# Attention, two MLPs and Sinkhorn on one core: 1/|p|^2 transposed instead of conj(p)/|p|^2, with the order around it

## The reference

```python
scale = np.minimum(mag, 0.999) / (mag + 1e-06)
new_re = ar * S_re - ai * S_im
new_im = ar * S_im + ai * S_re
S_re, S_im = (new_re + k_t outer v_t, new_im)
y_t = q_t @ S_re
```

## Time and profile before

| what | value |
|---|---|
| median of 3 runs | 2314.96 us (2314.71 to 2316.58) |
| the profiled execution, its own time | 2314.06 us |
| its span, first to last instruction | 2312.3 us |
| TensorE busy | 2228.5 us (96%) |
| VectorE busy | 1736.3 us (75%) |
| ScalarE busy | 1000.8 us (43%) |
| GpSimd busy | 506.5 us (22%) |
| mean granted TensorE clock | 0.990 |

### The profile page before, as it was taken

One profiled execution on the slowest core, in us unless ns is written; L12 is line 12 of the kernel. 1 busy time (PEld: TensorE's weight loads), 2 busy tenths in 40 slices (PEclk: granted clock), 3 DMA queues, 4 the chain that ended last, 5 costly groups with the idle time before them and its releaser, 6 DMA issues.

```text
span 2312.3 us, 38147 instructions
## 1 busy us (share of the span) xinstructions
PE 2228.5 (96%) x13735; PEld 2080.2 (90%) x13735; DVE 1736.3 (75%) x3033; ACT 1000.8 (43%) x1689; POOL 506.5 (22%) x332
## 2 busy tenths in 40 slices
PE   3799999999998989999999999999999999999999
PEld 2799999999998889999998899999998999999998
DVE  7888888888855777677777777777778777776775
ACT  3565666556555424333344333443334333344332
POOL 0000000000000333222332223322323223332222
PEclk9899999999999999999999999999999999999999
DMA  4211111111103121111011230111111211011111
GB/s 122 83 49 50 53 50 49 50 50 49 43 29 123 42 82 56 55 55 55 31 51 55 83 107 30 55 55 55 55 42 41 82 56 55 29 53 54 54 55 28
DMA packets 70726, 131.34 MB, mean 57 GB/s; under 512 B 5512, under 2 KB 36488, under 8 KB 70536
## 3 DMA queue, kind: packets, MB, share of 16 engines
q1 hardware_dynamic: 70536, 129.14, 17.2%
HBM read 114.96 MB, written 14.16 MB: 56 GB/s over the span
## 4 chain that ended last, share of the span: by engine, by line
PE 88%; DVE 8%; issue 1%; ACT 1%; DMA 0%; POOL 0%; SPq 0%; DVEq 0%; ACTq 0%
PE bank L1536 15%; PE bank L1537 15%; PE bank L1538 15%; PE bank L1701 11%; PE bank L1702 11%; PE bank L1703 11%; PE bank L1485 2%; PE bank L1504 2%; PE bank L1514 2%; PE bank L1513 2%; PE bank L1471 1%; PE bank L1523 1%; DVE tmp L923 1%; DVE u_s L1319 1%; DVE x_raw L1215 0%
## 5 line engine op out<-in xcount | busy, mean ns | idle before, releaser
L1701 PE MATMUL bank<-w_h,h_h 128*128 128x384 f32 x1536 | 516.0, 336 | 11.2 <-DVE acc L1345 6.8
L1703 PE MATMUL bank<-w_h,h_l 128*128 128x384 f32 x1536 | 514.1, 335 | 0.0
L1702 PE MATMUL bank<-w_l,h_h 128*128 128x384 f32 x1536 | 514.0, 335 | 0.0
L597 POOL TENSOR_TENSOR h_l<-u_s,h_h 128x512 fp32r<-128x512 f32 x192 | 245.1, 1298 | 974.8 <-ACT h_h L830 974.8
L1537 PE MATMUL bank<-x_l,w_h 128*128 128x512 f32 x1056 | 414.4, 392 | 0.0
L1536 PE MATMUL bank<-x_h,w_h 128*128 128x512 f32 x1056 | 414.2, 392 | 0.0
L1538 PE MATMUL bank<-x_h,w_l 128*128 128x512 f32 x1056 | 413.3, 391 | 0.0
L1345 DVE SCALAR_TENSOR_TENSOR acc<-bank,prob,acc 128x384 f32<-128x384 f32 x352 | 214.5, 612 | 174.2 <-PE bank L1703 171.5
L1701 PEld LDWEIGHTS bank<-w_h,h_h 128*128 128x128 f32 x1536 | 288.9, 188 | 17.2 <-DVE acc L1345 10.0
L1702 PEld LDWEIGHTS bank<-w_l,h_h 128*128 128x128 f32 x1536 | 288.9, 188 | 2.0
L1703 PEld LDWEIGHTS bank<-w_h,h_l 128*128 128x128 f32 x1536 | 288.8, 188 | 0.0
(11 more groups left out here) (176 smaller groups left out, 4133.6 us busy)
## 6 DMA issues: line engine op xcount, KB each, us to landing
...
```

The lines of the kernel that those rows point to most:

```text
L597: pool.tensor_tensor(tiles_of(h_l, name), group_sum(name), tiles_of(h_h, name).bitcast(F32), ALU.subtract).then_inc(hl_done, 1)
L1701: pe.matmul(dst, h_h[:, f, t_], w2h[:, fw], start=n == 0, stop=False)
L1702: pe.matmul(dst, h_h[:, f, t_], w2l[:, fw], start=False, stop=False)
L1703: mm = pe.matmul(dst, h_l[:, f, t_], w2h[:, fw], start=False, stop=n == 3)
```

## The change

Instead of p * rr, two parts, the kernel now takes `rr` alone to tokens: `r_by_tokens` has the small product and three transposes, into att[2]. On DVE `k_by_r` multiplies the transposed rr by k into the new tile `kr` and `by_k` multiplies kr by the transposed p, which stays in att[0] and att[1]. `pre_inv` (POOL) and `first_inv` (DVE) go. In odd units `r_by_tokens` stands directly behind `p_by_tokens`, ahead of `tile_in(t)`; in even units it stays behind `tile_in(t)`. The banks are passed round: q's transposes go to att[3] and att[2], k's to att[0] and att[1], the scores to att[3] and att[2], y to att[0]. `ACT.p_root` now waits for `r_there`, `state_sum` always follows `y_sum`, `ysum` has two columns so that ACT may run one unit ahead, and SP loads the next k after `k_by_r`. In the tail, x2_hi and x2_lo of the last group but one move ahead of `g_hi` / `g_lo` of round m = 2, the first expert's weight work moves from rounds 1 and 2 to rounds 2 and 3, and TensorE runs the first expert's first product `p1_0` ahead of the last `mm_out`.

```diff
@@ -59,7 +59,7 @@
 R_MAX = 2.0 ** 80
-R_ONE = 2.0 ** 60
+R_ONE, R_HALF = 2.0 ** 60, 2.0 ** 30
 P2_MIN = 2.0 ** -93
@@ -125,7 +125,7 @@
         yr = sb("yr", [128, KT, 128], F32, ab)
-        ysum = sb("ysum", [128, 1], F32, ab)
+        ysum = sb("ysum", [128, 2], F32, ab)
         an = sb("an", [128, 2, NI, BKJ], F32, ab)
@@ -134,7 +134,7 @@
         rr = sb("rr", [128, KT, 128], F32, ab)
-        pinv = sb("pinv", [128, 2, KT, 128], F32, ab)
+        kr = sb("kr", [128, DM], F32, ab)
         qb = sb("qb", [128, DM], F32, ab)
@@ -149,7 +149,7 @@
         prod = tmp2[:].rearrange("p r k t -> p (r k t)")[:, 0:4 * BKJ].rearrange("p (q r n) -> p q r n", q=2, r=2)
-        mask_rows = pinv[:, 0, 0]
+        mask_rows = kr[:, 0:128]
@@ -331,7 +332,7 @@
                 if u:
-                    sp.wait_ge(k_mul, 2 * u)
+                    sp.wait_ge(kr_done, u)
                 sp.dma_start(kb[:], permuted(k[u // B, u % B])).then_inc(k_in, 16)
@@ -484,12 +485,6 @@
             pool.memset(inv_b[:], -1.0).then_inc(filled, 1)
-            def pre_inv(u):
-                pool.wait_ge(r_done, u + 1)
-                pool.wait_ge(i_there, 2 * u)
-                pool.tensor_tensor(pinv[:], p[:], rr[:].unsqueeze(1).to_broadcast([128, 2, KT, 128]), ALU.mult)\
-                    .then_inc(pinv_done, 1)
@@ -574,8 +569,6 @@
                 check_y(u)
-                if 2 <= u + 1 < UNITS:
-                    pre_inv(u + 1)
@@ -641,9 +634,9 @@
-                if u:
-                    act.wait_ge(floor_done, u)
-                act.activation(sq[:, 1], yr_u[:], ACT.Square, scale=2.0 ** -22, accum_out=ysum[:]).then_inc(ysq_done, 1)
+                if u > 1:
+                    act.wait_ge(floor_done, u - 1)
+                act.activation(sq[:, 1], yr_u[:], ACT.Square, scale=2.0 ** -22, accum_out=ysum[:, u % 2:u % 2 + 1]).then_inc(ysq_done, 1)
@@ -652,23 +645,23 @@
                 if u:
-                    act.wait_ge(pinv_done, u)
+                    act.wait_ge(r_there, u)
                     act.wait_ge(last_done, u)
...
             def stacks(u, half):
-                there, done, dst = ((qt_there, qs_done, qs), (kt_there, ks_done, ks))[half]
+                there, done, dst, from_ = ((qt_there, qs_done, qs, (3, 2)), (kt_there, ks_done, ks, (0, 1)))[half]
                 for n in range(2):
...
                     act.activation(dst[0:96, 4 * n:4 * n + 4],
-                                   att[2 * half + n][0:96, :].rearrange("p (h t) -> p h t", h=4), ACT.Copy)\
+                                   att[from_[n]][0:96, :].rearrange("p (h t) -> p h t", h=4), ACT.Copy)\
                        .then_inc(done, 1)
...
                 act.wait_ge(y_there, u + 1)
-                act.activation(y, att[2][:, 0:DM], ACT.Copy).then_inc(y_done, 1)
+                act.activation(y, att[0][:, 0:DM], ACT.Copy).then_inc(y_done, 1)
@@ -798,13 +791,15 @@
                 t = (GROUPS - 1) * TILES + m
+                if m == 2:
+                    x2_hi(GROUPS - 2)
                 g_hi(t - 1)
...
                 if m == 2:
-                    x2_hi(GROUPS - 2)
-                if m == 1:
-                    for part in range(3):
-                        w1_hi(0, 0, 0, part)
+                    w1_hi(0, 0, 0, 0)
+                    w1_hi(0, 0, 0, 1)
+                if m == 3:
+                    w1_hi(0, 0, 0, 2)
                 if m == 6:
@@ -907,7 +902,7 @@
                    .then_inc(scaling, 1)
-                dve.tensor_scalar(r_last[:, u % 4, KT:KT + 1], ysum[:], 2.0 ** 64, None, ALU.mult).then_inc(floor_done, 1)
+                dve.tensor_scalar(r_last[:, u % 4, KT:KT + 1], ysum[:, u % 2:u % 2 + 1], 2.0 ** 64, None, ALU.mult).then_inc(floor_done, 1)
                 dve.wait_ge(scaling, n + 3)
@@ -982,7 +977,6 @@
                     dve.wait_ge(p_there, 2 * u)
-                    dve.wait_ge(pinv_done, u)
                 dve.tensor_tensor(p[:, 0], tmp2[:, 0], tmp2[:, 1], ALU.subtract).then_inc(final_step, 1)
@@ -1006,18 +1000,8 @@
-            def first_inv(u):
-                dve.wait_ge(r_done, u + 1)
-                if u:
-                    dve.wait_ge(i_there, 2 * u)
-                else:
-                    dve.wait_ge(mask_done, 1)
-                dve.tensor_tensor(pinv[:], p[:], rr[:].unsqueeze(1).to_broadcast([128, 2, KT, 128]), ALU.mult)\
-                   .then_inc(pinv_done, 1)
             def bound(u):
-                dve.wait_ge(i_there, 2 * u + 1)
+                dve.wait_ge(r_there, u + 1)
                 dve.tensor_reduce(r_sum[0:1, u:u + 1], att[2][0:1, DM:DM + KT + 1], AX.X, ALU.add).then_inc(bound_done, 1)
@@ -1027,26 +1011,30 @@
-            def by_k(u, parts=(0, 1)):
+            def k_by_r(u):
+                bound(u)
                 dve.wait_ge(k_in, 16 * (u + 1))
-                for n in parts:
-                    if n == 0:
-                        bound(u)
-                    dve.wait_ge(i_there, 2 * u + n + 1)
-                    dve.scalar_tensor_tensor(kt[:, :, n], att[2 + n][:, 0:DM].rearrange("p (h d) -> p h d", h=H), -R_ONE,
-                                             kb[:].rearrange("p (h d) -> p h d", h=H), ALU.mult, ALU.mult)\
+                if u == 0:
+                    dve.wait_ge(mask_done, 1)
+                dve.scalar_tensor_tensor(kr[:], att[2][:, 0:DM], -R_HALF, kb[:], ALU.mult, ALU.mult).then_inc(kr_done, 1)
+            def by_k(u):
+                dve.wait_ge(kr_done, u + 1)
+                for n in range(2):
+                    dve.scalar_tensor_tensor(kt[:, :, n], att[n][:, 0:DM].rearrange("p (h d) -> p h d", h=H), R_HALF,
+                                             kr[:].rearrange("p (h d) -> p h d", h=H), ALU.mult, ALU.mult)\
                        .then_inc(k_mul, 1)
...
                     dve.wait_ge(s_there, 2 * u + n + 1)
-                    dve.tensor_tensor(at[:, 4 * n:4 * n + 4], att[n][:].rearrange("p (h t) -> p h t", h=4),
+                    dve.tensor_tensor(at[:, 4 * n:4 * n + 4], att[3 - n][:].rearrange("p (h t) -> p h t", h=4),
                                       mask[:].unsqueeze(1).to_broadcast([128, 4, 128]), ALU.mult).then_inc(at_done, 1)
...
                 dve.wait_ge(st_there, u + 1)
-                dve.wait_ge(y_there, u + 1)
                 dve.tensor_tensor(state[0:96, b, 0:DM], att[3][0:96, 0:DM], state[0:96, b, 0:DM], ALU.add)\
@@ -1088,16 +1076,14 @@
                 p_inv(0)
-                first_inv(0)
                 scale_sum(2)
-                by_k(0, (0,))
+                k_by_r(0)
+                by_k(0)
                 final(1)
-                by_k(0, (1,))
                 p_sum(1)
...
                 p_inv(1)
-                first_inv(1)
                 scale_sum(3)
@@ -1106,9 +1092,10 @@
                 by_q(1)
-                blocks(1, 1, 3)
+                blocks(1, 1, 2)
+                k_by_r(1)
                 by_k(1)
-                blocks(1, 3, NI)
+                blocks(1, 2, NI)
                 masked(1)
@@ -1150,6 +1137,7 @@
                     blocks(pair, BLOCKS_AHEAD, BLOCKS_AHEAD + 1)
+                k_by_r(u)
                 by_k(u)
@@ -1281,15 +1269,15 @@
                 t = (GROUPS - 1) * TILES + m
-                g_lo(t - 1)
                 if m == 2:
                     x2_lo(GROUPS - 2)
+                g_lo(t - 1)
                 if m == 5:
...
                 g_max(t)
-                if m == 1:
+                if m == 2:
                     w1_sums(0, 0, 0)
-                if m == 2:
+                if m == 3:
                     w1_lo(0, 0)
@@ -1454,46 +1442,45 @@
         def _(pe):
-            def to_tokens(u, src, done, first_bank):
+            def p_by_tokens(u):
+                pe.wait_ge(p_done, u + 1)
                 for n in range(2):
-                    if first_bank == 2 and n == 0:
-                        if u:
-                            pe.wait_ge(xl_done, u)
-                        pe.wait_ge(last_done, u + 1)
-                        pe.wait_ge(floor_done, u + 1)
-                        pe.matmul(att[2][:, DM:DM + KT + 1], ones[:], r_last[:, u % 4], start=True, stop=True)
-                    if first_bank == 2 and n == 1 and u:
-                        pe.wait_ge(state_done, u)
                     for kk in range(KT):
-                        mm = pe.transpose(att[first_bank + n][:, kk * 128:(kk + 1) * 128], src[:, n, kk], ident[:])
-                    mm.then_inc(done, 1)
-            def p_by_tokens(u):
-                pe.wait_ge(p_done, u + 1)
-                to_tokens(u, p, p_there, 0)
-            def inverse_by_tokens(u):
-                pe.wait_ge(pinv_done, u + 1)
-                to_tokens(u, pinv, i_there, 2)
-            def by_channels(src, done, first_bank):
-                for m in range(2):
-                    for n in range(4):
-                        mm = pe.transpose(att[first_bank + m][0:96, n * 128:(n + 1) * 128],
```

(60 more changed lines are left out.)

11 lines of the change are left out of this document (6 added, 5 removed).

## The result

The changed kernel took **2303.52 us** (median of 5 runs, 2300.98 to 2304.72) against 2314.92 for the kernel before (5 runs, 2314.40 to 2316.58). The ratio is 0.9947, 95% interval 0.9933 to 0.9961: faster by 11.4 us. I had predicted 2294.9, range 2290 to 2302. The sign was right, the gain about half of what I gave, and the time lies outside the range. The profiled execution took 2301.36 us, its span is 2299.6, 12.7 less than before (2312.3).

What follows compares the result with a forecast made beforehand. TensorE was taken to bound from about 145 to 714 us, VectorE's chain before that. Terms 4.2 + 6.6 + 7.3 + 2.0 = 20.1 us off 2314.06 gave 2294.0, as median 2294.9; range 2290 to 2302.

Steps and rivals of the forecast that it cites:

- The start: Units 0 to 4, up to q_and_k(4): 141.7 against 145.91, 4.2 us earlier, bounds -1.5 and -6.7.
- The TensorE-bound units: Units 5 to 23: three transposes fewer (0.30 each) and one switch less in odd units, 6.6 us, bounds 5.5 and 7.
- the term that failed: Unit 1: y_sum 5.5 us after idle TensorE, then state_sum 1.4; state added at 73.3 instead of 71.97, +1.4 us.
- unit 4: TensorE arrives at 139.05 against 141.28; without the 2.53 wait its rate stays full, mm_out 2.2 instead of 3.46 us.
- The mask of unit 0: VectorE in unit 0: the mask moves from 47.49 to 45.0, with the first pinv gone and k's products earlier.
- rival 3: VectorE becomes the bound in the middle, its 11 us of added k work visible: 2306 us; chance 0.09.
- rival 4: Odd units stall on bank 2, r_by_tokens(u) waiting for x_lo(u - 1): slower, 2333 us; chance 0.04.
- the switch: Odd units 5 to 23: one switch less from transposes to fp32r products, 0.09 us each.
- the page's rule: Transposes don't engage the full clock; three fewer would save about 0.66 us each time, some 14 us; the prediction weighed against it.
- The tail: Wait of 4.65 us for x2's low half and slow rate behind it go, 7.3 us; last mm_out 2.0 us.
- rival 2: Tail's wait moves: g_lo of round 3 behind w1_lo comes after mm_in wants it; 2299 us; chance 0.14.
- Rival 1: Clock stays up in units 0 and 1, y_sum 3.8 us twice, first units give up to 6.7: 2292.4 us; chance 0.2.

Runs made afterwards that it cites:

- the spare products: Changed kernel with 16 products that nobody reads ahead of y_sum in units 0 and 1, order kept: 2296.64 us, ratio 0.9922 to the kernel before.
- all of the start: Changed kernel with state_sum first, 12 and 8 unread products, final(2) ahead of state_add(1), unit 3's r_by_tokens behind its first tile: 2293.48 us, ratio 0.9909 to before.
- the order put back: Changed kernel with state_sum ahead of y_sum in units 0 and 1, in a bank of its own: 2297.82 us, ratio 0.9931 to the kernel before.

## Why the prediction was wrong in size

The start was to give 4.2 us and cost 1.2: 5.4 of the 7.7 us that are missing in the account. None of my rivals had a start that becomes longer. The TensorE-bound units are 2.2 us short.

**Unit 1, and through it the first units: the term that failed.** I had called it my least certain and gave +1.4 us to the addition of the state; it is +4.8. Three estimates were each too small. The mask of unit 1 came at 66.20, not 65.05, since the state of unit 0 was itself added at 55.24 and not at 54.2. `y_sum(1)` took 6.44 us, not 5.5. And I took 1.4 us for `state_sum`, its price at full clock; behind the slow `y_sum` it ran slow too, 2.56 us in unit 1 and 2.04 in unit 0. Together 1.15 + 0.94 + 1.16 = 3.25 of the 3.4 us. My upper bound for `y_sum`, 7.6 at half rate throughout, held; the value between did not. I had averaged between "full" and "half", where both units ran at the low level (1.2 GHz) for nearly the whole of it.

**Units 2 and 3, not in the sum.** `y_sum(2)` too runs slow, 5.85 us behind 2.40 us of idle time. Of the 2.2 us over its full rate only about 1.0 reach the path, since up to unit 4 the chain runs over VectorE. There they show as a wait for the transposes of p(3), which has no counterpart before:

```profile
115.08 1.02 DVE L1011 TENSOR_TENSOR qt<-bank,qb 128x384 f32<-128x384 f32 x2 [0.97 <-PE bank L1450]
```

The second execution of the same kernel shows it without a change of code: `y_sum(2)` at 3.65, no such wait, and from the addition of state 1 to the first product of unit 4 66.63 us instead of 67.63 (66.60 with the spare products). The variant with all of the start paid 1.05 at p(23) for the same thing. Another 0.7 went in unit 2: of the 1.05 us that VectorE gained by the end of `pinv`, a wait for ScalarE's `g_h` took 0.7 back at once (1.37 us ahead of `g_l` at 106.72, where it had been 0.67). 3.4, 1.0 and 0.7 are 5.1 of the 5.4 us that are missing at `q_and_k(4)`.

**What the change gained in the start is real.** The waits for GpSimd are gone, and unit 4 went as I had it: a wait of 0.34 us in place of 2.53, and 2.21 us for the `mm_out` behind it instead of 3.46. The mask of unit 0 is at 44.73 (I said 45.0), and a weight subtraction in unit 2 takes 0.95 us where one took 2.00 beside `pinv`:

```profile
103.32 0.95 DVE L1073 TENSOR_TENSOR w_in_l<-w_in_raw,w_in_h 128x768 fp32r<-128x768 f32 x1
```

The scores of unit 4 start at 151.76 in the kernel before, at 153.10 in the changed one, and at 148.66 with the order put back: -3.1 for the rest of the change, three quarters of the -4.2 that I had given to the whole start. The order swallowed that and more.

On the weight subtraction: the Trainium skill, "SBUF — State Buffer", section "SBUF: two separate sides", says that VectorE and GpSimd share one pair of ports which one of them holds for a whole instruction while the other is blocked; for VectorE that holds, by the page, of an instruction with two inputs in SBUF, as this subtraction is, beside a GpSimd instruction that reads SBUF. The two rows agree: 0.95 us without GpSimd, and 2.00 beside its 1.82, ending 0.81 us behind it.

**The TensorE-bound units: right in kind, 2.2 us too large.** TensorE stays at 100%, VectorE does not become the bound (rival 3 is out), no odd unit stalls on bank 2 (rival 4 is out). A pair of units is 0.50 us shorter; I had 0.69. Three transposes fewer are 0.33 us (0.61 to 0.28), a little more than my 0.30, and the small product of even units fell from 0.23 to 0.14. Against that the tiles give back 0.19 in each even unit, and the 0.09 for the switch is nothing. Counting one kind of instruction is not enough where the duration of its neighbours hangs on it.

On the page's rule against which I weighed this term: in the changed kernel three transposes take 0.28 us at a granted clock of 1.00, and 0.67 in unit 2, behind the wait of 6.02, so they follow the clock, as I read it from the earlier trace rows. The Trainium skill, "TensorE: Matmul & The Clock Gate", part 4, says that they don't; the runs speak against it. (By the prediction's own 0.66 that rule gives 19 x 0.66 + 0.9 = 13.4 us, not 14.)

**The tail: right.** 9.56 us measured with unit 23's transposes in it, 9.3 alone, by the two mechanisms named; rival 2 (the wait moves to g_lo of round 3) is out.

**Rival 1** (the clock stays up in units 0 and 1) was the wrong way round in this kernel, but shows what was to be had: with the clock kept up by spare products the time is 2296.6; I had given 2292.4 for it. Of the 4.2 us between, 2.7 are there at `q_and_k(4)`, 141.91 where 6.7 us of gain would be 139.2: the spare products held `y_sum(1)` back by about 3. About 2 more are the TensorE-bound units.

The range failed with it: its ends came from bounds of terms (13.0 to 23.6 us together), but the bad end for the start, -1.5, held a slow `y_sum` in unit 1 alone, with `state_sum` at full rate and units 2 and 3 as they were; and the TensorE-bound units, at 4.0, fell short of their own lower bound of 5.5 (5.1 up to p(23)).
